# Layer 1's first product by seven products instead of eight, for two thirds of the tokens

## The chip, the core and the metric

One NeuronCore of one Trainium2 chip runs the whole program. Its engines are PE (TensorE, matrix products), DVE (VectorE), ACT (ScalarE), POOL (GpSimd) and SP, which here only issues DMA. The metric is the device time of one execution in microseconds (us); the median of several runs counts.

## The reference, cut to what matters

```python
# q, k, v: 4 x 8 heads x 576 x 64, fp32; Dmat: causal decay by head
ret = (q @ k.T / 8) * Dmat;  x = (ret @ v), rearranged to 2304 x 512
# layer 1: w_in 512 x 2048, w_out 2048 x 512
h = x @ w_in
g = np.where(h >= 1, h, np.where(h <= -1, 0, (h + 1) ** 2 / 4))
x = g @ w_out
# layer 2: w_a, w_b 512 x 1536, w_out 1536 x 512
out = ((x @ w_a) * (x @ w_b)) @ w_out
```

## The kernel before

Every fp32 operand x of the two layers is split in two: high = x rounded to the matrix engine's format by an ACT copy, low = x - high on DVE. A product is then three matmuls (high*high, high*low, low*high). Tokens are always along the free axis of `x_all` (4 blocks of 128 features x 2304 tokens), which stays in SBUF.

**Attention** (16 units of two heads) runs first and fills `x_all`. It is the only part in which POOL works.

**Layer 1** goes through the tokens in five tiles t of 512, 512, 256, 512 and 512 tokens (`WIDTHS`), and in each through 16 blocks f of 128 hidden features. `hidden(t, f)` is 12 matmuls (4 input blocks x 3) into a PSUM bank, and `project(t, f)` 12 more, which add the block's share of w_out to four banks `y_b`; PE runs `hidden(f)`, `project(f - 2)`. Between them stands `gate`: ACT takes two relus from PSUM (L893, L895), DVE adds and multiplies (L717, L720), ACT rounds (`gh`, L904), DVE takes the low part (`gl`, L726). The weights' split is made in tile 0 (`round_w1`, `split_w1`), three blocks ahead. In tiles 1 to 4, after the gates that `prep_steps` names, DVE and ACT also prepare layer 2's weights: four sums of 256 columns (`block_sums`), the rounding of seven operands (`round_ops`, L840 of 768 columns and L842 of 1,024) and their low parts (`split_ops`, L657, L660). SP stores them to DRAM, 12 blocks in all.

**Layer 2** has three tiles of 768 tokens with 12 steps u each. A step computes blocks of a = x w_a and b = x w_b by Strassen's scheme in Winograd's form: seven products of half-size operands instead of eight. A product is 6 matmuls of 384 columns. PE's order in a step (`step2`) is: product 1, product 2, product 7 of the step before, `rows` (three half-shares of the product with w_out, 6 matmuls of 512 columns each, from step 5 on), product 5, product 4 of the step before, product 6, product 3. ACT and DVE copy and add the products in between (u1, a0, b1, p5, u2, a1), DVE multiplies (`prod1`, and `prod0` once product 4 is done, L781), ACT rounds (`ph`, L946 and L957) and DVE takes low parts (`pl`). Product 1 of step u + 1 reuses the bank that `prod0` of step u - 1 has read, and so waits for `prod0_ready`, and for the step's weights, which SP loads into one of three buffers `wop` when product 4 of three steps before is done.

Every engine works through its own list in the written order; a semaphore wait holds all that stands behind it on that engine.

## Time and profile before

| | us |
|---|---|
| median of 3 runs | 881.57 (881.54 to 882.55) |
| the profiled execution | 882.61 |
| its span, first to last instruction | 880.1 |
| PE busy | 870.2 (99%) |
| DVE busy | 479.8 (55%) |
| ACT busy | 334.6 (38%) |
| POOL busy | 37.0 (4%), all in the attention part |
| granted TensorE clock, mean | 1.00 of full speed |

The profiled execution is 1.04 us above the median, and 2.5 us of it lie outside the span. Layer 1 starts on PE at 67.3 us of the span, layer 2's first product at 461.6 us. A matmul's busy time (390 ns for 512 columns) is longer than the distance to the next one (227 ns), since they are pipelined; how fast PE gets on is read from start to start.

### The profile page before, as it was taken

How to read it: one execution, taken by the hardware profiler on the slowest of the kernel's cores; microseconds unless marked ns; L12 is line 12 of the kernel's file. 1: busy time of each engine (PE TensorE's matmuls, PEld its weight loads, DVE VectorE, ACT ScalarE, POOL GpSimd, SP SyncE). 2: the span in 40 equal slices, each digit the busy share in tenths (PEclk: the TensorE clock that was granted, in tenths of full speed). 3: DMA queues.
4: the chain of work that ended last, by engine and by line, in shares of the span. 5: the costliest groups of instructions: out<-in, count | busy, mean ns of one | idle time of the engine just before them, and what ended most of it. 6: DMA issues, size and time to landing. Idle time of an engine off the chain costs nothing.

```text
span 880.1 us, 13001 instructions
## 1 busy us (share of the span) xinstructions
PE 870.2 (99%) x5232; PEld 777.0 (88%) x5232; DVE 479.8 (55%) x829; ACT 334.6 (38%) x598; POOL 37.0 (4%) x54
## 2 busy tenths in 40 slices
PE   7999999999999999999999999999999999999998
PEld 6998888888899888888889999999999999999996
DVE  4686665555656755665653533574433574534443
ACT  1235554444445544444443333342233242223220
POOL 4660000000000000000000000000000000000000
PEclk9999999999999999999999999999999999999999
...
GB/s 344 329 348 264 1 0 1 79 111 116 111 123 108 54 107 119 111 112 105 118 149 189 243 168 184 198 157 200 150 198 157 284 159 215 168 216 168 227 60 72
DMA packets 33451, 136.89 MB, mean 156 GB/s; under 512 B 2672, under 2 KB 13424, under 8 KB 28784
## 3 DMA queue, kind: packets, MB, share of 16 engines
...
q10 hardware_dynamic: 144, 0.20, 0.1%
...
## 4 chain that ended last, share of the span: by engine, by line
PE 97%; DMA 1%; SPq 1%; DVE 0%; ACT 0%; issue 0%; POOL 0%; POOLq 0%; DVEq 0%; ACTq 0%
PE score_b L523 6%; PE score_b L527 6%; PE score_b L525 6%; PE score_a L527 4%; PE score_a L523 4%; PE score_a L525 4%; PE score_a L477 4%; PE kv_b L494 4%; PE kv_b L496 4%; PE score_a L479 4%; PE ret_b L496 4%; PE score_b L479 4%; PE score_a L478 4%; PE kv_b L495 4%; PE score_b L477 4%; PE ret_b L495 4%
## 5 line engine op out<-in xcount | busy, mean ns | idle before, releaser
L717 DVE TENSOR_TENSOR gate_w<-relu_s,relu_r 128x512 f32<-128x512 f32 (+1 forms) x80 | 51.0, 638 | 97.2 <-ACT relu_r L895 97.1
L523 PE MATMUL score_b<-xop_hi,wop 128*128 128x384 f32 x288 | 96.8, 336 | 0.1
L527 PE MATMUL score_b<-xop_hi,wop 128*128 128x384 f32 x288 | 96.7, 336 | 0.0
L525 PE MATMUL score_b<-xop_lo,wop 128*128 128x384 f32 x288 | 96.5, 335 | 0.0
L904 ACT ACTIVATE gh<-gated 128x512 fp32r<-128x512 f32 (+1 forms) x80 | 47.2, 590 | 105.9 <-DVE gated L720 105.9
L726 DVE TENSOR_TENSOR gl<-gated,gh 128x512 fp32r<-128x512 f32 (+1 forms) x80 | 51.1, 639 | 50.8 <-ACT gh L904 50.6
L523 PE MATMUL score_a<-xop_hi,wop 128*128 128x384 f32 x216 | 72.2, 334 | 0.0
L527 PE MATMUL score_a<-xop_hi,wop 128*128 128x384 f32 x216 | 72.2, 334 | 0.0
L525 PE MATMUL score_a<-xop_lo,wop 128*128 128x384 f32 x216 | 72.2, 334 | 0.0
L954 ACT ACTIVATE p<-score_b 128x384 f32<-128x384 f32 x36 | 17.7, 490 | 105.3 <-PE score_b L527 105.3
L523 PEld LDWEIGHTS score_b<-xop_hi,wop 128*128 128x128 f32 x288 | 54.1, 188 | 2.0 <-ACT p L954 0.4
L946 ACT ACTIVATE ph<-prod 128x384 fp32r<-128x384 f32 x36 | 18.9, 526 | 96.4 <-DVE prod L763 96.4
L525 PEld LDWEIGHTS score_b<-xop_lo,wop 128*128 128x128 f32 x288 | 54.1, 188 | 1.3
L527 PEld LDWEIGHTS score_b<-xop_hi,wop 128*128 128x128 f32 x288 | 54.0, 188 | 0.0
L720 DVE SCALAR_TENSOR_TENSOR gated<-relu_s,gate_w 128x512 f32<-128x512 f32 (+1 forms) x80 | 51.1, 638 | 2.7
L781 DVE TENSOR_TENSOR prod<-score_a,a 128x384 f32<-128x384 f32 x18 | 10.0, 557 | 72.6 <-PE score_a L527 72.6
L893 ACT ACTIVATE relu_s<-score_a,half 128x512 f32<-128x512 f32 (+1 forms) x40 | 25.8, 646 | 55.4 <-PE score_a L479 55.4
L781 DVE TENSOR_TENSOR prod<-score_b,a 128x384 f32<-128x384 f32 x18 | 10.0, 557 | 64.5 <-PE score_b L527 64.5
L477 PE MATMUL score_a<-xh,w1a 128*128 128x512 f32 (+1 forms) x120 | 44.4, 370 | 0.0
L478 PE MATMUL score_a<-xl,w1a 128*128 128x512 f32 (+1 forms) x120 | 44.2, 368 | 0.0
L479 PE MATMUL score_a<-xh,w1a 128*128 128x512 f32 (+1 forms) x120 | 44.1, 368 | 0.0
L548 PE MATMUL kv_b<-wo_hi,pl 128*128 128x512 f32 x112 | 43.9, 392 | 0.0
...
## 6 DMA issues: line engine op xcount, KB each, us to landing
...
```

The costliest lines, as they stand in the source:

```text
L477: pe.matmul(o, w1_slab(f, 0)[:, at], xh[:, k, 0:WIDTHS[t]], start=(k == 0), stop=False)
L478: pe.matmul(o, w1_slab(f, 0)[:, at], xl[:, k, 0:WIDTHS[t]], start=False, stop=False)
L479: mm = pe.matmul(o, w1_slab(f, 1)[:, at], xh[:, k, 0:WIDTHS[t]], start=False, stop=(k == KT - 1))
L495: pe.matmul(o, w1_slab(f, 0)[:, at], gl[:, f % RING, 0:WIDTHS[t]], start=False, stop=False)
L496: mm = pe.matmul(o, w1_slab(f, 1)[:, at], gh[:, f % RING, 0:WIDTHS[t]], start=False, stop=(f == NF1 - 1))
L523: pe.matmul(o, w[:, 0, at], xop_hi[b][:, k, :], start=(start and k == 0), stop=False, skip_group_check=True)
L525: pe.matmul(o, w[:, 0, at], xop_lo[b][:, k, :], start=False, stop=False, skip_group_check=True)
L527: mm = pe.matmul(o, w[:, 1, at], xop_hi[b][:, k, :], start=False, stop=(k == 1), skip_group_check=True)
L717: nc.vector.tensor_tensor(gate_w[:, 0:WIDTHS[t]], relu_s[:, 0:WIDTHS[t]], relu_r[:, 0:WIDTHS[t]], ALU.add).then_inc(gatew_ready, 1)
L720: nc.vector.scalar_tensor_tensor(out=gated[:, 0:WIDTHS[t]], in0=relu_s[:, 0:WIDTHS[t]], scalar=1.0, in1=gate_w[:, 0:WIDTHS[t]], op0=ALU.mi ...
L726: nc.vector.tensor_tensor(gl[:, f % RING, 0:WIDTHS[t]], gated[:, 0:WIDTHS[t]], raw(gh[:, f % RING, 0:WIDTHS[t]]), ALU.subtract).then_inc(g ...
L904: nc.scalar.activation(gh[:, f % RING, 0:WIDTHS[t]], gated[:, 0:WIDTHS[t]], ACT.Copy).then_inc(gh_ready, 1)
```

## The change: what it does

- Layer 1's tokens 0 to 767 are still done by `hidden` and `project`, now in two tiles of 384 (`TC = 384`). The other 1,536 tokens form two tiles of 768, which run through the Strassen steps: a step v takes two of the 16 hidden blocks, so there are 8 steps a tile, v = 0 to 15. Layer 2 follows as steps v = 16 to 51 (u = v - 16).
- In such a step the four results a0, a1, b1 and the last main bank are hidden features before the gate. `gate_relu` (ACT) takes s = relu(h/2 + 1/2), `gate_sum` (DVE, two instructions) takes max(h, min(s, 1) s), `gate_high` (ACT) rounds, `low_parts` (POOL) takes the low part. There are four of each a step. The buffer `u_sum` serves both u1 and u2.
- The product with w_out is made of `chunk`s: 12 matmuls of 384 columns, four of them in one row in each of steps 3 to 18, between product 7 and product 5; DVE adds each to `x_all` (ACT copies the first of a tile).
- In layer 1's two ordinary tiles SP stores all split weights to DRAM (`store_slabs`), loads pairs of blocks once more (`load_s`), POOL makes the four sums, ACT and DVE split them after the gates in `prep_steps`, SP stores them (`store_s`). Steps 0 to 15 load their operands from there, and w_out's split.
- Layer 2's weights are no longer prepared in layer 1. In its first tile (u = 0 to 11) the operands of step u + 1 are made during step u in the buffer `wop` itself: POOL sums, `round_ops(u + 1, 0)` and `(u + 1, 1)` on ACT, `split_ops` on DVE. PE's product 1 waits for `op_lo_ready`, that is for both parts. SP stores them for the later tiles.

Three places in the engines' lists. First PE between steps 2 and 3 of layer 2 (products 3 and 1; product 4 of the step before and product 6 stand right ahead of them). `score_b` holds product 3's bank and, for an odd step, the main bank. Before:

```order
L523 MATMUL score_b<-xop_hi,wop 128x384 [waits p5_copied]
L525 MATMUL score_b<-xop_lo,wop 128x384
L527 MATMUL score_b<-xop_hi,wop 128x384
L523 MATMUL score_b<-xop_hi,wop 128x384
L525 MATMUL score_b<-xop_lo,wop 128x384
L527 MATMUL score_b<-xop_hi,wop 128x384
L523 MATMUL score_b<-xop_hi,wop 128x384 [waits wop_loaded0,prod0_ready]
```

After:

```order
L684 MATMUL score_b<-xop_hi,wop 128x384 [waits p5_copied]
L686 MATMUL score_b<-xop_lo,wop 128x384
L688 MATMUL score_b<-xop_hi,wop 128x384
L684 MATMUL score_b<-xop_hi,wop 128x384
L686 MATMUL score_b<-xop_lo,wop 128x384
L688 MATMUL score_b<-xop_hi,wop 128x384
L684 MATMUL score_b<-xop_hi,wop 128x384 [waits op_lo_ready,prod0_ready]
```

The matmuls are the same; the last row, product 1, waits for DVE's low parts in place of a load.

Second ACT in step 2 of layer 2 (u, u_sum: copies of the main bank; p: of product 5; ph: the roundings of the step's results; wo_hi: those of w_out). Before:

```order
L932 ACTIVATE u<-score_a 128x384 [waits p1_done,a0_ready]
L946 ACTIVATE ph<-prod 128x384 [waits prod1_ready]
L954 ACTIVATE p<-score_b 128x384 [waits p5_done,b1_ready]
L957 ACTIVATE ph<-prod 128x384 [waits prod0_ready]
L862 ACTIVATE wo_hi<-wo_raw 128x512 [waits wo_loaded0] x2
L965 ACTIVATE u<-score_a 128x384 [waits p6_done,a1_ready]
```

After:

```order
L1199 ACTIVATE u_sum<-score_a 128x384 [waits p1_done,a1_ready]
L1059 ACTIVATE wop<-ab_raw 128x768 [waits ab_loaded,op_stored0,p4_done]
L1216 ACTIVATE ph<-prod 128x384 [waits prod1_ready,rows_done]
L1227 ACTIVATE p<-score_b 128x384 [waits p5_done,b1_ready]
L1233 ACTIVATE ph<-prod 128x384 [waits prod0_ready]
L1062 ACTIVATE wop<-wop_sum 128x1024 [waits sums_ready]
L1098 ACTIVATE wo_hi<-wo_raw 128x512 [waits wo_loaded0] x2
L1244 ACTIVATE u_sum<-score_a 128x384 [waits p6_done,a0_ready]
```

Two roundings for step 3 have come in, the second (L1062) behind the rounding that waits for `prod0_ready`.

Third ACT in step 1, the second step of the stage that uses Strassen's scheme: before that is layer 2's, now layer 1's (x_all: the last ordinary tile's results). Before:

```order
L932 ACTIVATE u<-score_b 128x384 [waits p1_done,a0_ready]
L946 ACTIVATE ph<-prod 128x384 [waits prod1_ready]
L884 ACTIVATE x_all<-kv_b 128x512 [waits xl_ready,y_done]
L884 ACTIVATE x_all<-kv_b 128x512
L954 ACTIVATE p<-score_b 128x384 [waits p5_done,b1_ready]
```

After:

```order
L1199 ACTIVATE u_sum<-score_b 128x384 [waits p1_done,a1_ready]
L1182 ACTIVATE ph<-a_0 128x384 [waits g_ready]
L1182 ACTIVATE ph<-a 128x384 [waits g_ready]
L1173 ACTIVATE prod<-b,half 128x384 [waits g_ready,b1_ready]
L1182 ACTIVATE ph<-b 128x384 [waits g_ready]
L1127 ACTIVATE x_all<-kv_b 128x384 [waits xl_ready,y_done]
L1127 ACTIVATE x_all<-kv_b 128x384
L1227 ACTIVATE p<-score_b 128x384 [waits p5_done,b1_ready]
```

Three gate roundings and a relu stand ahead of the copy of product 5 (L1227), for which product 3 waits.

The diff, cut to its core:

```diff
-        prep_steps = {(1, 1): 0, (1, 5): 1, (1, 9): 2, (1, 13): 3, (2, 2): 4, (2, 8): 5,
-                      (3, 1): 6, (3, 5): 7, (3, 9): 8, (3, 13): 9, (4, 1): 10, (4, 5): 11}
+        prep_steps = {(0, 10): 0, (0, 12): 1, (0, 14): 2, (1, 0): 3, (1, 2): 4, (1, 4): 5, (1, 6): 6,
+                      (1, 8): 7}
+            for p in range(NF1 // 2):
+                load_s(p)
+                store_slabs(p)
+                if p:
+                    store_s(p - 1)
+            store_s(NF1 // 2 - 1)
+            for v in range(WBUF):
+                load_ops(v)
+            load_out1(0)
+            load_out1(1)
...
+            def store_slabs(p):
+                for f in (2 * p, 2 * p + 1):
+                    sp.wait_ge(w1_ready, f + 1)
+                    sp.dma_start(w1_outs[f // GROUP, :, :, f % GROUP, :],
+                                 raw(w1_all[f][:, :, DM:])).then_inc(slabs_stored, 16)
+                sp.dma_start(w1_ops[p, :, :, 0:2 * AW],
+                             raw(w1_all[2 * p][:, :, 0:2 * AW])).then_inc(slabs_stored, 16)
+                sp.dma_start(w1_ops[p, :, :, 2 * AW:3 * AW],
+                             raw(w1_all[2 * p + 1][:, :, AW:2 * AW])).then_inc(slabs_stored, 16)
+            def store_s(p):
+                sp.wait_ge(s_lo_ready, p + 1)
+                sp.dma_start(w1_ops[p, :, :, 3 * AW:], raw(s_op[p % 2][:, :, :])).then_inc(s_stored[p % 2], 16)
...
+            def load_ab(u):
+                if u:
+                    sp.wait_ge(op_lo_ready, 2 * u - 1)
+                    sp.wait_ge(sums_ready, 4 * u)
+                sp.dma_start(ab_raw[:, :], w2_ab[u]).then_inc(ab_loaded, 16)
+            def store_ops(u):
+                sp.wait_ge(op_lo_ready, 2 * u + 2)
+                sp.dma_start(w2_ops[u], raw(wop[(V1 + u) % WBUF][:, :, :])).then_inc(op_stored[u % WBUF], 16)
...
+            def sums(a11, a12, a21, a22, s1, s2, s3, s4, ready, n):
+                nc.gpsimd.tensor_tensor(s1, a21, a22, ALU.add).then_inc(ready, 1)
+                nc.gpsimd.tensor_tensor(s3, a11, a21, ALU.subtract).then_inc(ready, 1)
+                pool.wait_ge(ready, 4 * n + 1)
+                nc.gpsimd.tensor_tensor(s2, s1, a11, ALU.subtract).then_inc(ready, 1)
+                pool.wait_ge(ready, 4 * n + 3)
+                nc.gpsimd.tensor_tensor(s4, a12, s2, ALU.subtract).then_inc(ready, 1)
+            for p in range(NF1 // 2):
+                pool.wait_ge(s_loaded[p % 2], 16 * (p // 2 + 1))
+                a, o = s_raw[p % 2], s_sum[p % 2]
+                sums(a[:, 0, 0:AW], a[:, 0, AW:], a[:, 1, 0:AW], a[:, 1, AW:],
+                     *[o[:, i * AW:(i + 1) * AW] for i in range(4)], s_sums_ready, p)
+            def second_sums(u):
+                v = V1 + u
+                a11, a12, a22, a21 = [ab_raw[:, i * AW:(i + 1) * AW] for i in range(4)]
+                o = wop_sum[v % WBUF]
+                sums(a11, a12, a21, a22, *[o[:, (3 + i) * AW:(4 + i) * AW] for i in range(4)], sums_ready, u)
+            def low_parts(p, i):
+                half, row = [(0, 0), (1, 0), (1, 1), (0, 1)][i]
+                g = [a0[p % 2], a1, b1, prod1][i]
+                at, half = (2 * p + row) % GBUF, slice(half * HALF, (half + 1) * HALF)
+                pool.wait_ge(gh1_ready, 4 * p + i + 1)
+                nc.gpsimd.tensor_tensor(pl[at][:, half], g[:, :], raw(ph[at][:, half]),
+                                        ALU.subtract).then_inc(gl1_ready, 1)
+            for v in range(1, V1 + NF2):
+                if v <= V1:
+                    low_parts(v - 1, 0)
+                    low_parts(v - 1, 1)
+                if 0 <= v + 1 - V1 < NF2:
+                    second_sums(v + 1 - V1)
+                if v <= V1:
+                    low_parts(v - 1, 2)
+                    low_parts(v - 1, 3)
...
+                q, half, m = n // 8, n // 4 % 2, n % 4
+                pe.wait_ge(gl1_ready, 8 * q + 8)
+                pe.wait_ge(wo_loaded[q % 2], 32 * (q // 2 + 1))
+                if n < 4:
+                    pe.wait_ge(y_copied, KT * NT)
+                else:
+                    pe.wait_ge(rows_out[n % 4], n // 4)
+                o, at, tokens = y_b[n % 4][:, 0:HALF], slice(m * P, (m + 1) * P), slice(half * HALF, (half + 1) * HALF)
+                for i in range(GROUP):
+                    hi, lo = ph[(GROUP * q + i) % GBUF][:, tokens], pl[(GROUP * q + i) % GBUF][:, tokens]
+                    w_hi, w_lo = wo_hi[q % 2][:, i, at], wo_lo[q % 2][:, i, at]
+                    pe.matmul(o, w_hi, hi, start=(i == 0), stop=False)
+                    pe.matmul(o, w_hi, lo, start=False, stop=False)
+                    mm = pe.matmul(o, w_lo, hi, start=False, stop=(i == GROUP - 1))
+                mm.then_inc(rows_done, 1)
...
+                    if 0 <= u < NF2:
+                        pe.wait_ge(op_lo_ready, 2 * u + 2)
+                    else:
+                        pe.wait_ge(wop_loaded[v % WBUF], 16 * loads_of(v))
+                    product(1, v, main_b[v % 2], True).then_inc(p1_done, 1)
...
-                    pe.wait_ge(u2_copied, u)
-                    product(7, u - 1, main_b[(u - 1) % 2], False).then_inc(p7_done, 1)
-                for n, half in mine:
-                    rows(n, half)
-                if u < STEPS2:
-                    if u == 0:
+                    pe.wait_ge(u2_copied, v)
+                    product(7, v - 1, main_b[(v - 1) % 2], False).then_inc(p7_done, 1)
+                for n in chunks(v):
+                    chunk(n)
+                if u >= 0:
+                    for n, half in slots(u):
+                        rows(n, half)
...
+                    pe.wait_ge(u1_copied, v + 1)
+                    product(6, v, main_b[v % 2], False).then_inc(p6_done, 1)
+                    pe.wait_ge(p5_copied, v + 1)
+                    product(3, v, p5_b, False).then_inc(p3_done, 1)
...
+            def gate_sum(p, i):
+                s = [prod1, prod0, prod0, prod1][i]
+                h = [a0[p % 2][:, :], a1[:, :], b1[:, :], main_b[p % 2]][i]
+                o = [a0[p % 2], a1, b1, prod1][i]
+                dve.wait_ge(s_ready, 4 * p + i + 1)
+                nc.vector.scalar_tensor_tensor(out=s[:, :], in0=s[:, :], scalar=1.0, in1=s[:, :], op0=ALU.min,
+                                               op1=ALU.mult).then_inc(v_ready, 1)
+                dve.wait_ge(v_ready, 4 * p + i + 1)
+                nc.vector.tensor_tensor(o[:, :], h, s[:, :], ALU.max).then_inc(g_ready, 1)
...
+                if 0 <= u + 1 < NF2:
+                    split_ops(u + 1, 0)
+                move(v, 1)
+                add_chunks(v)
+                if u >= 0:
+                    add_rows(u, 0)
+                if gated_before:
+                    gate_sum(v - 1, 3)
+                elif v:
                     g = (u - 1) % GBUF
-                    dve.wait_ge(p4_done, u)
-                    nc.vector.tensor_tensor(prod0[:, :], main_b[(u - 1) % 2], a0[(u - 1) % 2][:, :],
+                    dve.wait_ge(p4_done, v)
+                    nc.vector.tensor_tensor(prod0[:, :], main_b[(v - 1) % 2], a0[(v - 1) % 2][:, :],
                                             ALU.mult).then_inc(prod0_ready, 1)
...
+                if 0 <= u + 1 < NF2:
+                    split_ops(u + 1, 1)
...
+            def round_ops(u, part):
+                v = V1 + u
+                o = wop[v % WBUF]
+                if part == 0:
+                    act.wait_ge(p4_done, v - WBUF + 1)
+                    if u >= WBUF:
+                        act.wait_ge(op_stored[u % WBUF], 16 * (u // WBUF))
+                    act.wait_ge(ab_loaded, 16 * (u + 1))
+                    nc.scalar.activation(o[:, 0, 0:3 * AW], ab_raw[:, 0:3 * AW], ACT.Copy).then_inc(op_hi_ready, 1)
+                else:
+                    act.wait_ge(sums_ready, 4 * u + 4)
+                    nc.scalar.activation(o[:, 0, 3 * AW:], wop_sum[v % WBUF][:, 3 * AW:],
+                                         ACT.Copy).then_inc(op_hi_ready, 1)
...
+            def gate_relu(p, i):
+                s = [prod1, prod0, prod0, prod1][i]
+                h = [a0[p % 2][:, :], a1[:, :], b1[:, :], main_b[p % 2]][i]
+                act.wait_ge([a0_ready, a1_ready, b1_ready, p4_done][i], p + 1)
+                if p and i < 2:
+                    act.wait_ge(gl1_ready, 4 * p)
+                elif i >= 2:
+                    act.wait_ge(g_ready, 4 * p + 2)
+                    if i == 3:
+                        act.wait_ge(gl1_ready, 4 * p)
+                nc.scalar.activation(s[:, :], h, ACT.Relu, bias=half[:, 0:1], scale=0.5).then_inc(s_ready, 1)
+            def gate_high(p, i):
+                half, row = [(0, 0), (1, 0), (1, 1), (0, 1)][i]
+                g = [a0[p % 2], a1, b1, prod1][i]
+                if p >= 4:
+                    act.wait_ge(rows_done, 8 * ((p - 4) // 2) + 8)
+                act.wait_ge(g_ready, 4 * p + i + 1)
+                nc.scalar.activation(ph[(2 * p + row) % GBUF][:, half * HALF:(half + 1) * HALF], g[:, :],
+                                     ACT.Copy).then_inc(gh1_ready, 1)
...
-                        act.wait_ge(a0_ready, u)
+                if gated_before:
+                    gate_relu(v - 1, 0)
+                    gate_relu(v - 1, 1)
+                if v < V:
+                    if v:
+                        act.wait_ge(a1_ready, v)
+                    act.wait_ge(p1_done, v + 1)
+                    nc.scalar.activation(u_sum[:, :], main_b[v % 2], ACT.Copy).then_inc(u1_copied, 1)
+                if gated_before:
+                    gate_high(v - 1, 0)
+                    gate_high(v - 1, 1)
+                if 0 <= u + 1 < NF2:
+                    round_ops(u + 1, 0)
+                if gated_before:
+                    gate_relu(v - 1, 2)
+                    gate_high(v - 1, 2)
...
+                if v < V:
+                    if v:
+                if gated_before:
+                    gate_relu(v - 1, 3)
+                    gate_high(v - 1, 3)
+                elif v:
                     act.wait_ge(prod0_ready, u)
                     nc.scalar.activation(ph[g][:, 0:HALF], prod0[:, :], ACT.Copy).then_inc(ph0_ready, 1)
-                    for v in outs_split(u):
-                if moving and f == 0:
-                    round_op(nxt, 6)
-            for u in range(STEPS2 + 1):
-                step2(u)
+                if 0 <= u + 1 < NF2:
+                    round_ops(u + 1, 1)
+                if u > 0:
+                    for w in outs_split(u):
+                        round_out(w)
+                if u >= 0:
+                    copy_rows(u, 1)
```

## Rows read from the trace of the kernel before

**Rows 1.** The page: busy time and instructions; the chain that ended last, by engine.
```profile
PE 870.2 (99%) x5232; PEld 777.0 (88%) x5232; DVE 479.8 (55%) x829; ACT 334.6 (38%) x598; POOL 37.0 (4%) x54
...
PE 97%; DMA 1%; SPq 1%; DVE 0%; ACT 0%; issue 0%; POOL 0%; POOLq 0%; DVEq 0%; ACTq 0%
```

**Rows 2.** Timeline of PE, layer 1: start us, us, line, operation.
```profile
80.59 0.39 PE L477 MATMUL score_b<-xh,w1a 128*128 128x512 f32 x1
...
83.31 0.39 PE L494 MATMUL kv_b<-gh,w1a 128*128 128x512 f32 x1
```

**Rows 3.** Timeline of PE, layer 2, around the end of product 4 of a step.
```profile
621.68 0.33 PE L523 MATMUL score_a<-xop_hi,wop 128*128 128x384 f32 x1
...
622.55 0.33 PE L527 MATMUL score_a<-xop_hi,wop 128*128 128x384 f32 x1
...
623.76 0.33 PE L523 MATMUL score_b<-xop_hi,wop 128*128 128x384 f32 x1
...
624.80 0.33 PE L523 MATMUL score_a<-xop_hi,wop 128*128 128x384 f32 x1
```

**Rows 4.** Timeline of DVE at the same place.
```profile
622.92 0.56 DVE L781 TENSOR_TENSOR prod<-score_a,a 128x384 f32<-128x384 f32 x1 [4.92 <-PE score_a L527]
```

**Rows 5.** Timeline of ACT at the same place.
```profile
623.52 0.53 ACT L957 ACTIVATE ph<-prod 128x384 fp32r<-128x384 f32 x1 [1.08 <-DVE prod L781]
623.95 0.62 ACT L862 ACTIVATE wo_hi<-wo_raw 128x512 fp32r<-128x512 f32 x1
```

**Rows 6.** Groups by line and shape, DVE: xcount, busy us, mean ns, idle before.
```profile
L720 DVE SCALAR_TENSOR_TENSOR gated<-relu_s,gate_w 128x512 f32<-128x512 f32 x64 | 44.3, 692 | 2.2
...
L792 DVE TENSOR_TENSOR a<-score_b,u 128x384 f32<-128x384 f32 x36 | 19.9, 553 | 13.1 <-PE score_b L527 12.6 <-ACT u L965 0.5
...
L660 DVE TENSOR_TENSOR op_lo<-op_sum,op_hi 128x1024 fp32r<-128x1024 f32 x12 | 14.7, 1226 | 0.0
...
L720 DVE SCALAR_TENSOR_TENSOR gated<-relu_s,gate_w 128x256 f32<-128x256 f32 x16 | 6.8, 425 | 0.5
```

**Rows 7.** Groups by line and shape, ACT.
```profile
L893 ACT ACTIVATE relu_s<-score_a,half 128x512 f32<-128x512 f32 x32 | 22.1, 690 | 51.5 <-PE score_a L479 51.5
...
L946 ACT ACTIVATE ph<-prod 128x384 fp32r<-128x384 f32 x36 | 18.9, 526 | 96.4 <-DVE prod L763 96.4
...
L842 ACT ACTIVATE op_hi<-op_sum 128x1024 fp32r<-128x1024 f32 x12 | 12.5, 1043 | 0.0
...
L893 ACT ACTIVATE relu_s<-score_a,half 128x256 f32<-128x256 f32 x8 | 3.8, 469 | 3.9 <-PE score_a L479 3.9
```

**Rows 8.** Timeline of PE, second step of layer 2 (step 1).
```profile
475.67 0.34 PE L527 MATMUL score_b<-xop_hi,wop 128*128 128x384 f32 x1
476.10 0.44 PE L523 MATMUL score_b<-xop_hi,wop 128*128 128x384 f32 x1
476.38 0.33 PE L525 MATMUL score_b<-xop_lo,wop 128*128 128x384 f32 x1
```

**Rows 9.** Timeline of ACT at the same place.
```profile
475.56 0.49 ACT L954 ACTIVATE p<-score_b 128x384 f32<-128x384 f32 x1
```

**Rows 10.** Timeline of POOL in the attention part.
```profile
44.90 0.86 POOL L396 TENSOR_TENSOR qd<-kq,decays 128x384 f32<-128x384 f32 x1 [1.44 <-PE ret_b L459]
...
63.51 1.70 POOL L396 TENSOR_TENSOR qd<-kq,decays 128x384 f32<-128x384 f32 x1 [1.12 <-PE ret_b L459]
65.17 0.30 POOL L400 TENSOR_TENSOR qd<-kq,decays 128x64 f32<-128x64 f32 x1
```

**Rows 11.** Timeline of DVE at the same place.
```profile
63.26 1.23 DVE L638 TENSOR_TENSOR w1a<-w1a_raw,w1a 128x1024 fp32r<-128x1024 f32 x1 [0.27 <-ACT w1a L834]
```

**Rows 12.** Window of layer 1: us, busy by engine, PE clock, DMA share, GB/s.
```profile
195.00:200.00 5.00, 5.00 (x23) 4.14 (x23) 1.64 (x4) 1.90 (x3) 0.00 (x0) 1.00 0.87 359
```

**Rows 13.** Windows at the start of layer 2.
```profile
472.00:474.00 2.00, 2.00 (x14) 2.00 (x13) 1.48 (x3) 0.00 (x0) 0.00 (x0) 1.00 0.99 377
...
478.00:480.00 2.00, 2.00 (x13) 2.00 (x12) 0.94 (x3) 0.49 (x1) 0.00 (x0) 1.00 0.99 423
```

494 lines of the change are left out of this document (280 added, 214 removed).

## The prediction

> **What bounds the kernel now.** I read the busy times first: PE is busy for 99% of the span, DVE for 55%, ACT for 38%, and the chain that ended last is 97% PE [rows 1]. So the kernel lasts as long as PE's list, and whatever makes PE wait is added in full. Next the starts of matmuls. In layer 1, 12 matmuls of 512 columns take from 80.59 to 83.31, 226.7 ns each [rows 2]; in layer 2, 12 of 384 columns take from 621.68 to 623.76, 173.3 ns each [rows 3]. The difference is 53.4 ns for 128 columns, 0.417 ns a column, which is the clock's upper level of 2.4 GHz; what stays is 13.3 ns for each matmul, whatever its width. A matmul of 256 columns then costs 120.0 ns. Last I looked at the joints, the places where PE goes on with what another engine has just made. The change puts new work into them. The joint that matters is the one from product 4 to the next product 1, with products 6 and 3 in between: product 4's last matmul starts at 622.55 and ends at t0 = 622.88, product 1 starts at 624.80, that is t0 + 1.92 [rows 3]. Until then PE needs nothing. DVE starts `prod0` 0.04 after t0 [rows 4], ACT rounds it 0.04 after its end and is free for its next operation at 623.95, t0 + 1.07 [rows 5]. Nothing waits there now. One joint of before does fail, in step 1: ACT ends the copy of product 5 at 476.05 [rows 9], PE's stream, due at 475.84, goes on with 476.10 and 476.38 [rows 8]. Its second matmul stands as if the first had started at 476.21, so from an engine's end to PE's stream it is 0.16, and that place costs 0.37.
>
> **The matmuls.** Before, layer 1 has 16 blocks x 24 matmuls x 5 tiles = 1,920: 1,536 x 0.2267 + 384 x 0.1200 = 394.3 us. After: two tiles of 384 columns, 768 matmuls; 16 steps x 42 for the seven products, 672; 64 chunks x 12, 768. That is 2,208 x 0.1733 = 382.7 us. The seven products save an eighth of the first product, 96 matmuls of 384 columns on 1,536 tokens, 16.6 us; the narrower matmuls give back 5. The stream gets shorter by **11.5 us**. Layer 2's and attention's matmuls stay.
>
> The Trainium skill ("TensorE: Matmul & The Clock Gate", Back-to-back issue gap) gives the distance of isolated matmuls at the upper clock as columns / 2.4 plus 2.5 ns; by that the narrower matmuls would give back only 0.7 us and the stream would shrink by 15.9 (an estimate from that page). The rows have 13.3 ns in place of 2.5, and they decide.
>
> **The joints of layer 2's first tile.** Here the operands of step u + 1 are made during step u. ACT's second rounding (1,024 columns, as L842: 1.04 us [rows 7]) stands behind the rounding of `prod0`, which waits for product 4. DVE's low part (as L660: 1.23 [rows 6]) waits for it, and product 1 waits for that. From t0: ACT is free at 1.07 [rows 5], rounds to 2.11, DVE from 2.15 to 3.38, PE goes on at 3.54. It wanted to at 1.92: a wait of 1.62. Nothing covers it, since between product 4 and product 1 PE has only products 6 and 3; rows and chunks stand ahead of product 4. Steps u + 1 = 2 to 11 have this joint: **10 x 1.62 = 16.2 us**.
>
> Steps 0 and 1 of layer 2 follow gates of layer 1, so the chain starts with the fourth gate: relu 384 columns wide (between 690 ns for 512 and 469 for 256 [rows 7]: 0.58), min-and-square (between 692 and 425 [rows 6]: 0.56), max (as an addition from PSUM, L792: 0.55 [rows 6]), each with a hop of 0.04: gate ready at t0 + 1.82. ACT rounds it (0.53 [rows 7]) and is free after 0.43, at 2.29, rounds the operands to 3.33, DVE ends at 4.60, PE goes on at 4.76. Wait 2.84, **2 x 2.84 = 5.7 us**.
>
> **The joints of layer 1's steps.** Product 1 of steps 4 to 15 waits only for the fourth gate: 1.82 + 0.16 = 1.98 against 1.92, 12 x 0.06 = **0.7 us**. Everything else of these steps (four relus, four roundings, three copies on ACT; fourteen or fifteen operations of about 0.55 us on DVE) has the four chunks to hide behind, 48 x 0.1733 = 8.3 us.
>
> Steps 1 and 2 have no chunks, only 7.3 us of matmuls each. In step 1 ACT reaches the copy of product 5 only after three gate roundings, a relu that waits for b1, and the copies of the last ordinary tile. Laid out with the durations above, b1 ends 3.9 us after the step's first matmul; the relu ends at 4.5. POOL's low part holds DVE's square until 4.7, max ends at 5.9, the rounding at 6.4, the two copies at 7.2, product 5's copy at 7.7. Product 3 was due at 6.2 and starts at 7.8: 1.6. The fourth gate then comes 0.65 too late for product 1. In step 2 the first relu waits for POOL's last low part of step 1, b1 is 1.05 late for product 4, product 5's copy 0.8 for product 3, the fourth gate 0.65 for product 1. Together **4.75 us**; from below I bound it by what the same place cost before, 0.4, from above by 8.2, if the four POOL operations of step 2, 0.86 each, hold DVE one after another. The 0.4 of before goes.
>
> **POOL.** A subtraction of 384 columns with both inputs in SBUF takes 0.86, one of 64 columns 0.30 [rows 10], so a sum of 256 about 0.65. POOL's work on layer 1's low parts hides behind the chunks; the sums of layer 2's operands for step u + 2 start at t0 and last 2.7. They collide: at 63.51 the same 0.86 operation took 1.70, and its end lies 0.72 after that of the 1,024-wide DVE subtraction that had started before it [rows 10, 11]. The reverse, DVE held by POOL, no row shows. It costs nothing at the least and one sum of 0.65 per joint at the most, 0 to 6.5 us over ten joints. I take 0.2 each, **2.0 us**, nearer to nothing, since only POOL's delay is in the rows.
>
> The rule for this is in the Trainium skill ("SBUF — State Buffer", Who interferes with whom): a DVE instruction with two SBUF inputs and a GpSimd instruction that reads SBUF exclude each other, and the one that started second waits for all of the first. The trace agrees for POOL's side. By the rule DVE's low part at t0 + 2.15 meets POOL's third sum: that is the second rival.
>
> **DMA in the ordinary tiles.** A step there is 24 x 0.1733 = 4.16 us. From block 10 of tile 0 on, each pair of steps (8.3 us) brings 1.83 MB of stored slabs, 1.05 MB of stored sums and 0.52 MB to load, 3.4 MB in all. The queue moved 359 GB/s at a share of 0.87 while storing [rows 12] and 377 to 423 at 0.99 while loading [rows 13], so I take 390: 8.7 us a pair. The queue falls behind by 0.4 each time, and the last sums reach ACT about 1 us late. PE has two half-steps, 4 us, in hand between a hidden block and its gate's use. I take 0. ACT's and DVE's loop there (two relus, gate, rounding, weights) is 3.9 us against 4.16.
>
> **The sum.** 882.61 - 11.5 - 0.4 + 16.2 + 5.7 + 0.7 + 4.75 + 2.0 = 900.1 for an execution like the profiled one. Median 1.04 lower: **899.0 us**.
>
> **The rivals.**
> 1. Forecast, the rounding between product 4 and product 1 binds twelve times: 893 to 905. For it: the order of ACT's list and the missing slack in rows 3 to 5. Chance 0.62.
> 2. POOL holds DVE as well, at nearly every joint. The third sum ends at t0 + 2.6 instead of the low part's start at 2.15, 0.45 more for ten joints instead of 0.2, and 2 more in steps 1 and 2: 903.5. For it: rows 10 and 11, seen from the other side; against it: no row of before has DVE held by POOL. Chance 0.20.
> 3. The stores bind. At 300 GB/s, below every row, a pair takes 11.4 us, 3.1 more than its steps; over five pairs 15, less 4 in hand: 11 more, 910. It decides from about 350 GB/s down. For it: the stores are pieces of 1 to 4 KB, and those of rows 12 are 7 KB. Chance 0.11.
> 4. Faster than before. The low part of the operands is ready by t0 + 1.92 (ACT takes it ahead of `prod0`'s rounding, or the time of a 1,024-wide operation overlaps with its neighbour). Then 16.2, 5.7 and 2.0 go and 875 is left. It decides once both stages together take less than 0.7 us after ACT is free; they take 2.3. Chance 0.05.
> 5. Gains and losses cancel: 0.02.
>
> About 0.2% is what a measurement of this kernel can tell from no change. Slower 0.93, faster 0.05, the same 0.02. The likeliest case alone spans 893 to 905. The range takes in the second rival and the lower edge of the third, and leaves the fourth out: 890 to 911.
>
> **What would show it.** In the trace after: 12 gaps of PE ahead of product 1 in layer 2's first tile, two of about 2.8 us and ten of 1.6 to 2.1, released by DVE's operand low part; none in the second and third tile. PE's matmuls in layer 1 sum to 382.7. Gaps ahead of product 3 in step 1 and of products 4 and 3 in step 2. Wrong are the joints if those gaps are missing or DVE was done long before; wrong is the DMA term if PE waits at the end of tile 0 or in tile 1, or step 0 starts later than 201 us into the span; wrong is the POOL term if L841 is 1.2 us long in each of them and starts right at ACT's end.

## The result and the profile after

The changed kernel takes 910.31 us (median of four runs, 909.31 to 910.35) against 881.59 (881.54 to 882.55): ratio 1.032, 95% interval 1.0302 to 1.0338. Slower, inside the range of 890 to 911, 11.3 us above the forecast of 899.0. Its profiled execution is the 909.31, with a span of 907.5 against 880.1; the other three took 1.0 us more, with spans of 908.5.

The page of the changed kernel, parts 1, 2 and 4, answers to [rows 1]:

```profile
PE 868.0 (96%) x5520; PEld 828.0 (91%) x5520; DVE 516.9 (57%) x873; ACT 348.0 (38%) x650; POOL 185.4 (20%) x198
...
PEclk9999999999999999999899999999999999999999
...
PE 80%; DVE 11%; ACT 5%; issue 2%; DMA 1%; SPq 1%; POOL 0%; ACTq 0%; DVEq 0%; POOLq 0%
```

PE has 288 instructions more, as forecast (2,208 less 1,920 matmuls), and DVE and ACT now hold 16% of the chain that was 97% PE. To see where, I took every start of a matmul and subtracted the start before it and the distance that a matmul of its width needs in a full stream (226.7 ns for 512 columns, 173.3 for 384). Before, what stays is 1.2 us in the whole span. After, it is 40.3. The span grew by 27.4, so the stream of matmuls itself shrank by 39.1 - 27.4 = 11.7 us (forecast 11.5). The loss is in six places. "Slow matmuls" are those that start 320 ns apart instead of 173, at the lower clock (last section). In this table a wait counts with the 0.1 us by which the matmul behind it is late too; elsewhere waits stand without it.

| place | forecast, us | measured, us |
|---|---|---|
| products 1 of steps 18 to 27 (ten joints) | 16.2 + 2.0 for POOL | 17.9 |
| product 1 of step 17 | 2.84 | 2.9 |
| product 1 of step 16 | 2.84 | 5.6, and 2.6 of slow matmuls behind it |
| steps 1 and 2 | 4.75 | 3.2, and 1.7 of slow matmuls |
| steps 4 to 15 | 0.7 | 0.6 |
| border from ordinary tile 0 to tile 1 | 0 | 5.3 |

An ordinary joint, timeline of PE, ACT, DVE and POOL around 478 us (start, duration, engine and line, operation, in brackets the idle time before it and who ended it); it answers to [rows 3 to 5]:

```profile
478.06 0.34 PE L688 MATMUL score_b<-xop_hi,wop 128*128 128x384 f32 x1
479.83 0.41 PE L684 MATMUL score_a<-xop_hi,wop 128*128 128x384 f32 x1 [1.43 <-DVE wop L841]
...
477.38 1.04 ACT L1062 ACTIVATE wop<-wop_sum 128x1024 fp32r<-128x1024 f32 x1
...
478.46 1.23 DVE L841 TENSOR_TENSOR wop<-wop_sum,wop 128x1024 fp32r<-128x1024 f32 x1 [0.54 <-ACT wop L1062]
...
478.47 1.79 POOL L522 TENSOR_TENSOR wop_sum<-wop_sum,ab_raw 128x256 f32<-128x256 f32 x1
```

This is the chain that was laid out: ACT's rounding of 1,024 columns, DVE's low part, PE 0.14 after it. PE starts 1.60 us late; the forecast was 1.62. Here POOL's sum is the one that waits: it began 0.01 after DVE's 1.23 and took 1.79.

The joint into step 16, PE, ACT, DVE and POOL:

```profile
435.67 0.34 PE L688 MATMUL score_b<-xop_hi,wop 128*128 128x384 f32 x1
441.17 0.66 PE L684 MATMUL score_a<-xop_hi,wop 128*128 128x384 f32 x1 [5.16 <-issue]
...
433.96 0.58 ACT L1173 ACTIVATE prod<-score_a,half 128x384 f32<-128x384 f32 x1 [0.49 <-PE score_a L688]
438.34 0.52 ACT L1182 ACTIVATE ph<-prod 128x384 fp32r<-128x384 f32 x1 [3.79 <-DVE prod L947]
438.77 1.04 ACT L1062 ACTIVATE wop<-wop_sum 128x1024 fp32r<-128x1024 f32 x1
...
428.68 1.49 DVE L837 TENSOR_TENSOR wop<-ab_raw,wop 128x768 fp32r<-128x768 f32 x1
430.14 3.13 DVE L848 TENSOR_TENSOR xop_lo<-x_all,xop_hi 128x768 fp32r<-128x768 f32 x2
433.30 2.02 DVE L862 TENSOR_TENSOR x_all<-x_all 128x768 f32<-128x768 f32 x2
435.24 1.01 DVE L888 TENSOR_TENSOR x_all<-kv_b,x_all 128x384 f32<-128x384 f32 x2
436.18 1.01 DVE L888 TENSOR_TENSOR x_all<-ret_b,x_all 128x384 f32<-128x384 f32 x2
437.10 0.55 DVE L944 SCALAR_TENSOR_TENSOR prod<-prod 128x384 f32<-128x384 f32 x1
...
439.84 1.23 DVE L841 TENSOR_TENSOR wop<-wop_sum,wop 128x1024 fp32r<-128x1024 f32 x1 [1.60 <-ACT wop L1062]
...
430.73 1.73 POOL L551 TENSOR_TENSOR pl<-b,ph 128x384 fp32r<-128x384 f32 x1
```

The relu of the fourth gate is done at 434.54 and DVE takes it up at 437.10, 2.6 us later: it is still making the next tile's x operands and adding chunks. The chain that was laid out then follows (4.07 us from DVE's start to PE's, laid out 4.10), and PE's next matmul behind the one of 435.67 starts at 441.17, 5.3 us late. Part of DVE's queue is POOL's doing: the low parts of 768 columns take 1.49 and 3.13 for two beside POOL, where one alone takes 0.95. That is about 1.8 us of the 2.6, an estimate from these rows.

The border of the ordinary tiles, PE, then DVE, then POOL:

```profile
134.13 0.41 PE L638 MATMUL score_a<-xh,w1a 128*128 128x384 f32 x1 [2.65 <-DVE xl L818]
...
122.60 1.23 DVE L823 TENSOR_TENSOR w1b<-w1b_raw,w1b 128x1024 fp32r<-128x1024 f32 x1 [0.39 <-ACT w1b L1044]
123.75 1.76 DVE L829 TENSOR_TENSOR s_op<-s_sum,s_op 128x1024 fp32r<-128x1024 f32 x1
125.44 1.09 DVE L912 TENSOR_TENSOR gate_w<-relu_s,relu_r 128x384 f32<-128x384 f32 x1
126.56 0.97 DVE L915 SCALAR_TENSOR_TENSOR gated<-relu_s,gate_w 128x384 f32<-128x384 f32 x1
...
132.90 4.10 DVE L818 TENSOR_TENSOR xl<-x_all,xh 128x384 fp32r<-128x384 f32 x4
...
122.92 1.50 POOL L519 TENSOR_TENSOR s_sum<-s_raw 128x256 f32<-128x256 f32 x1 [30.21 <-DMA s_raw<-w]
124.39 1.72 POOL L520 TENSOR_TENSOR s_sum<-s_raw 128x256 f32<-128x256 f32 x1
```

DVE's operations of 1.23 and 0.55 us take 1.76, 1.09 and 0.97 beside POOL's sums, and the four low parts of x, beside the next pair's sums, 4.10 in all, where four in a row take 1.97 in run 7. That is the side of the collision that no row of before had: DVE held by POOL.

### The profile page after: what moved, and what is told of

Same layout as the page of the kernel before. It is cut to its first block, busy times and chain, and to the rows that moved or that the text cites. A ratio compares the mean times of both kernels' runs of the same rounds, so it can differ in the third digit from the quotient of the medians.

```text
span 907.5 us, 14103 instructions
## 1 busy us (share of the span) xinstructions
PE 868.0 (96%) x5520; PEld 828.0 (91%) x5520; DVE 516.9 (57%) x873; ACT 348.0 (38%) x650; POOL 185.4 (20%) x198
## 4 chain that ended last, share of the span: by engine, by line
PE 80%; DVE 11%; ACT 5%; issue 2%; DMA 1%; SPq 1%; POOL 0%; ACTq 0%; DVEq 0%; POOLq 0%
PE score_b L684 7%; PE score_b L688 7%; PE score_b L686 7%; PE score_a L684 6%; PE score_a L686 6%; PE score_a L688 6%; PE kv_b L724 3%; PE kv_b L725 3%; PE kv_b L723 3%; PE ret_b L724 3%; PE ret_b L725 3%; PE ret_b L723 3%; PE kv_b L705 2%; PE kv_b L707 2%; PE kv_b L706 2%; PE ret_b L707 2%
## 5 line engine op out<-in xcount | busy, mean ns | idle before, releaser
L684 PE MATMUL score_b<-xop_hi,wop 128*128 128x384 f32 x416 | 140.9, 339 | 12.6 <-DVE wop L841 10.7
L688 PE MATMUL score_b<-xop_hi,wop 128*128 128x384 f32 x416 | 140.0, 337 | 0.0
L686 PE MATMUL score_b<-xop_lo,wop 128*128 128x384 f32 x416 | 139.7, 336 | 0.0
L684 PE MATMUL score_a<-xop_hi,wop 128*128 128x384 f32 x312 | 106.7, 342 | 12.9 <-DVE wop L841 7.4
L688 PE MATMUL score_a<-xop_hi,wop 128*128 128x384 f32 x312 | 105.7, 339 | 0.0
L684 PEld LDWEIGHTS score_b<-xop_hi,wop 128*128 128x128 f32 x416 | 78.4, 189 | 17.4 <-issue 12.4
L1227 ACT ACTIVATE p<-score_b 128x384 f32<-128x384 f32 x52 | 25.5, 491 | 153.5 <-PE score_b L688 153.5
L688 PEld LDWEIGHTS score_b<-xop_hi,wop 128*128 128x128 f32 x416 | 78.3, 188 | 0.0
L944 DVE SCALAR_TENSOR_TENSOR prod<-prod 128x384 f32<-128x384 f32 x64 | 38.0, 594 | 65.0 <-ACT prod L1173 65.0
L684 PEld LDWEIGHTS score_a<-xop_hi,wop 128*128 128x128 f32 x312 | 59.5, 191 | 15.8 <-issue 14.3
L688 PEld LDWEIGHTS score_a<-xop_hi,wop 128*128 128x128 f32 x312 | 59.7, 191 | 0.0
L686 PEld LDWEIGHTS score_a<-xop_lo,wop 128*128 128x128 f32 x312 | 59.6, 191 | 0.0
L551 POOL TENSOR_TENSOR pl<-a,ph 128x384 fp32r<-128x384 f32 x32 | 35.5, 1128 | 84.4 <-ACT ph L1182 84.4
L961 DVE TENSOR_TENSOR a<-score_a,u_sum 128x384 f32<-128x384 f32 x52 | 28.9, 555 | 26.9 <-PE score_a L688 26.3
L724 PE MATMUL kv_b<-wo_lo,ph 128*128 128x512 f32 x112 | 43.9, 392 | 0.0
L848 DVE TENSOR_TENSOR xop_lo<-x_all,xop_hi 128x768 fp32r<-128x768 f32 x35 | 35.1, 1021 | 15.0 <-ACT xop_hi L1088 14.8
L723 PE MATMUL kv_b<-wo_hi,ph 128*128 128x512 f32 x112 | 43.6, 389 | 0.0
## 6 DMA issues: line engine op xcount, KB each, us to landing
wo_lo<-w_outs SPq DMA_DIRECT2D x8, 1024.0 KB, 11.7
```

The source lines that it names most:

```text
L551: nc.gpsimd.tensor_tensor(pl[at][:, half], g[:, :], raw(ph[at][:, half]), ALU.subtract).then_inc(gl1_ready, 1)
L684: pe.matmul(o, w[:, 0, at], xop_hi[b][:, k, :], start=(start and k == 0), stop=False, skip_group_check=True)
L686: pe.matmul(o, w[:, 0, at], xop_lo[b][:, k, :], start=False, stop=False, skip_group_check=True)
L688: mm = pe.matmul(o, w[:, 1, at], xop_hi[b][:, k, :], start=False, stop=(k == 1), skip_group_check=True)
L723: pe.matmul(o, hi, w_hi, start=(u % GROUP == 0), stop=False)
L724: pe.matmul(o, hi, w_lo, start=False, stop=False)
```

## The experiments

Ten kernels. "The change" is the kernel at 910.3; "border" is that of ordinary tiles 0 and 1; waits of PE are read off as above. The time of a single run stands without an interval; its span less its waits and slow matmuls is 866.8 to 868.1 us in all ten and 867.2 in the change, so the lists of waits account for the times. Runs 5 to 8 were timed beside one execution of the kernel before of 883.8 us, 2 us above its usual time, so between them and the change a difference of 1 or 2 us says nothing by itself, and the waits in the traces decide.

**1. Both second parts early.** `round_ops(u + 1, 1)` behind `round_ops(u + 1, 0)`, on DVE likewise.

```diff
                 if 0 <= u + 1 < NF2:
                     round_ops(u + 1, 0)
+                    round_ops(u + 1, 1)
...
-                if 0 <= u + 1 < NF2:
-                    round_ops(u + 1, 1)
```

> Both second-part operations of layer 2's operands (ACT's rounding of the four sums, DVE's low part of them) stand right behind those of the first part, ahead of the chunks and rows, instead of between product 4 and product 1. Theory A (the place in ACT's and DVE's lists makes the joints; the sums themselves are ready early in the step): the eleven gaps of 1.6 to 2.9 us ahead of product 1 go (17.9 + 2.9 us), the one into step 16 shrinks from 5.3 to about 3.7, since DVE's 1.15 us now stand ahead of the preparation of the next x operands there: about 888 us, 885 if the clock no longer falls behind that gap. Theory B (the sums of POOL or the load of ab_raw are what comes late): ACT waits at the new place, the copy of product 5 behind it is late, and PE waits at product 3 instead: 905 or more.

892.7 us (four runs, 892.3 to 893.5), 1.0124 of before (1.0107 to 1.0141). Of the waits into steps 17 to 27 one of 1.4 us is left (the fourth gate's, into step 17), so the place in the lists did make them. But into step 16 PE waits 6.3, and in step 19 product 3 waits 1.2. ACT in step 15:

```profile
425.31 0.84 ACT L1058 ACTIVATE wop<-ab_raw 128x768 fp32r<-128x768 f32 x1
429.62 1.06 ACT L1061 ACTIVATE wop<-wop_sum 128x1024 fp32r<-128x1024 f32 x1 [3.47 <-POOL wop_sum L524]
430.58 0.60 ACT L1172 ACTIVATE prod<-b,half 128x384 f32<-128x384 f32 x1
```

That is theory B in part, and why 888 was missed by 5 us: in six of the twelve steps ACT stands at POOL's sums for 1.4 to 3.5 us, and in three of them PE waits for it. In step 15 the third relu comes 4.6 us later than in the change (425.99). I had taken the sums to be ready early in every step.

**2. Only ACT's rounding early.**

> Only ACT's rounding is moved ahead, DVE's low part stays between product 4 and product 1. If the chain is the sum of both stages, as the prediction put it, ACT's 0.95 and the rounding of prod0 ahead of it go from the path and DVE's list is left: prod0, the low part of prod1, the low part of the operands end at t0 + 2.2, PE goes on at t0 + 2.35 against 1.92. Ten gaps of 0.4 us instead of 1.7, the one into step 17 about 1.2 instead of 2.9, the one into step 16 about 3.9: some 16 us less than the changed kernel, 894. If DVE alone is the bound, little changes (908); if ACT alone, the gaps vanish (888).

899.4 us. The ten ordinary joints fall into two kinds: five of 0.40 to 0.45, as worked out, and five of 1.2 to 1.5. One of each, DVE, then POOL beside the first:

```profile
493.09 1.76 DVE L841 TENSOR_TENSOR wop<-wop_sum,wop 128x1024 fp32r<-128x1024 f32 x1
...
501.61 1.22 DVE L841 TENSOR_TENSOR wop<-wop_sum,wop 128x1024 fp32r<-128x1024 f32 x1
...
492.70 1.06 POOL L520 TENSOR_TENSOR wop_sum<-ab_raw 128x256 f32<-128x256 f32 x1
493.73 1.70 POOL L522 TENSOR_TENSOR wop_sum<-wop_sum,ab_raw 128x256 f32<-128x256 f32 x1
```

With POOL's sums at its side the low part of prod1 takes 0.78 instead of 0.55 and the operands' 1.76 instead of 1.22: 0.8 us a joint, against 0.3 in the change. The rest of the 5 us above the expected 894 is in steps 16 and 17: PE waits 6.0 and 1.6 there, not 3.9 and 1.2, since ACT stands at POOL's sums as in run 1 (3.5 us in step 15).

**3. Step 15's preparation behind the gate.**

```diff
+            if v == V1 - 1:
+                return {0: [], 1: [(j + 1, "op", 1)],
+                        2: [(j + 1, "op", 2), (j + 1, "t", 2), (j + 1, "t", 4), (j + 1, "op", 3)]}[place]
```

> In step 15 the x operand 2 and the two last differences of the next tile are made behind the step's last sum instead of ahead of the fourth gate. Theory A (DVE's backlog of this preparation makes the gap into step 16 5.3 us instead of the forecast 2.8, and the clock falls because the gap is that long): DVE starts the fourth gate's min-and-square at ACT's end, the gap is 2.8 us, and the 2.8 us of slow matmuls behind it go: 905. Rival (POOL's and DVE's collision at 430 makes it): the gap stays over 4 us: 909.

909.4 us, not the expected 905. The wait into step 16 is 2.81 us, so DVE's queue made the rest of the 5.3. The rival as it was put falls: DVE's operations ahead of the gate are still held by POOL (1.49 and 1.44), yet the gate starts on time. But together with the preparation the run took away one operation that POOL had held (1.76), and what the preparation would cost without POOL no run shows. The slow matmuls didn't go either: 9 behind this wait, 10 each behind two later ones (2.85 and 2.00) and 9 at the border. Waits and slow matmuls together are 40.3 us in both profiles: 3.8 less at this place, 1.5 and 1.9 more at the two later waits, 0.4 more at the border.

**4. ACT's order in steps 1 and 2.** Product 5's copy and the fourth relu ahead of the third gate's rounding, the tile's copies at the end of step 1.

> In steps 1 and 2 ACT copies product 5 and does the fourth relu ahead of the third gate's rounding, and the copies of the last ordinary tile stand at the end of step 1. Theory A (ACT's order makes the gaps of step 1 and 2): the gaps ahead of products 3 and 1, 3.2 us in all, shrink to 0.5 or less, and with them goes the fall of the clock from 221.7 to 225.5 (1.9 us): about 905.5. Rival (b1 is late because POOL's low parts hold DVE): the gaps ahead of product 3 go, those ahead of product 1 stay at 0.5 each, and the clock falls all the same: 908.

908.2 us. The waits ahead of products 3 and 1 are gone in both steps. In step 2 one of 1.3 us stands ahead of product 4:

```profile
225.79 0.44 PE L684 MATMUL score_b<-xop_hi,wop 128*128 128x384 f32 x1 [1.13 <-DVE b L969]
```

The forecast had it (b1 1.05 late); in the change the slow matmuls stand in its place, in runs 1 to 3 it is there with 1.3. The slow matmuls of step 1 are missing too, but they are missing in runs 1 to 3, which have the same waits there, so this run doesn't show why they came.

**5. Second parts placed behind the sums,** with the edit of run 3. In steps 15 and 16 they stand behind the third gate's rounding, in the others, on ACT, behind the copy of product 5 and, on DVE, ahead of `prod0`.

```diff
                     nc.scalar.activation(p5[:, :], p5_b, ACT.Copy).then_inc(p5_copied, 1)
+                if 1 < u + 1 < NF2:
+                    round_ops(u + 1, 1)
```

> The second part of layer 2's operands is made where its sums have just come: in the two steps that follow gates of layer 1 behind the third gate's rounding, in the other ten behind the copy of product 5 (ACT) and ahead of prod0 (DVE). Step 15's preparation of the next x operands is cut as in the run before that moved it. The run with both early parts left three waits (6.3 us into step 16, 1.4 into step 17, 1.2 in step 19) and 2.5 us of slow matmuls. If they come from ACT standing at POOL's sums, too far ahead in its list, they go, and the first layer-2 tile has no wait over 0.5 us: 882. If the early place itself is what the gates can't bear (DVE's 1.15 us ahead of the fourth gate), the waits into steps 16 and 17 stay at 1 to 1.5: 885.

898.1 us, with 28.2 us of waits and slow matmuls against 23.2 in run 1. The wait into step 16 is 1.1, but product 3 of step 16 waits 2.1 and product 1 of step 17 2.7, and the ten ordinary joints are back with 0.4 to 1.1 each (6.7 us), now released by `prod0`:

```profile
502.68 0.44 PE L687 MATMUL score_a<-xop_hi,wop 128*128 128x384 f32 x1 [0.93 <-DVE prod L999]
...
500.93 1.23 DVE L844 TENSOR_TENSOR wop<-wop_sum,wop 128x1024 fp32r<-128x1024 f32 x1 [1.11 <-ACT wop L1067]
502.07 0.55 DVE L999 TENSOR_TENSOR prod<-score_a,a 128x384 f32<-128x384 f32 x1
```

The low part has only changed places with the work it delayed. Both theories of this run (882 and 885) were too simple.

**6. The third pair's sums a tile later.** `prep_steps = {(0, 10): 0, (0, 12): 1, (1, 1): 2, (1, 3): 3, ... (1, 11): 7}`.

> Only two pairs' sums are rounded and split in the first ordinary tile (blocks 10 and 12), the other six from block 1 of the second tile on. Theory P (the place: the third pair's rounding and low part stand on ACT and DVE directly ahead of the next tile's x): 2.1 us less ahead of the x tile's rounding, and the wait at the border, 2.8 us, shrinks to about 0.8; POOL's sums still meet DVE there, so the small waits behind it (1.5 us) and the one at the copies (0.9) stay in part: 3 us less, 907. Theory L (POOL's sums hold DVE, three operations of 0.6 to 1.2 us took 1.1 to 1.8): the border loses at least 4 us still: 909. Theory D (the DMA queue): no change: 910.

912.0 us. The border's wait falls from 2.81 to 0.86, as theory P has it. DVE's first operations there are as long as in the change, but the low parts of x, now ahead of the next pair's sums, take 2.50 for four instead of 4.10, so the place and the collision both moved. The later pairs now come late, and ACT stands at the stored slabs:

```profile
182.68 0.85 ACT L1087 ACTIVATE xop_hi<-x_all 128x768 fp32r<-128x768 f32 x1 [6.76 <-DMA w_ops<-w1b]
```

PE waits 3.3 us at 184, with 1.7 of slow matmuls behind it, and 1.2 at 204. Here, not in the change, the stores bind.

**7. POOL's sums 8 columns wide.**

```diff
+                if ready is s_sums_ready and n >= 2:
+                    a11, a12, a21, a22, s1, s2, s3, s4 = [t[:, 0:8] for t in (a11, a12, a21, a22, s1, s2, s3, s4)]
```

> POOL's four sums of pairs 2 to 7 of layer 1's operands are 8 columns wide instead of 256; ACT and DVE round and split a piece of x_all of the same size in their place. This kernel leaves these sums out of the result. Every wait, transfer and operation of the other engines stays. Theory L: DVE's operations at the border go back to 0.55 and 1.23 us and the four low parts of x from 1.02 to 0.55 each: the border costs under 1.5 us instead of 5.3: 906. Theory P: the first wait stays over 2 us, only the small ones go: 908.5. Theory D: nothing changes: 910.

906.4 us. DVE at the same place:

```profile
124.22 1.23 DVE L831 TENSOR_TENSOR s_op<-s_sum,s_op 128x1024 fp32r<-128x1024 f32 x1
125.38 0.55 DVE L915 TENSOR_TENSOR gate_w<-relu_s,relu_r 128x384 f32<-128x384 f32 x1
125.96 0.56 DVE L918 SCALAR_TENSOR_TENSOR gated<-relu_s,gate_w 128x384 f32<-128x384 f32 x1
...
131.88 1.97 DVE L820 TENSOR_TENSOR xl<-x_all,xh 128x384 fp32r<-128x384 f32 x4
```

Every duration is back, and the border costs one wait of 0.7 us instead of 5.3 in all. The number and order of all operations, the sizes of those on ACT and DVE, and the transfers are the same. In the change ACT doesn't stand at the third pair's sums either (they end at 128.1, its rounding starts at 130.7), so it isn't their earlier end that helps here. Theory L holds.

**8. Thin stores.**

```diff
+                    wide = DM if f < GROUP else 8
                     sp.dma_start(w1_outs[f // GROUP, :, :, f % GROUP, 0:wide],
```

> The stores of W_out's rounded slabs are 8 columns wide from the fifth slab on, and the seven-product stage loads the first four slabs each time: 0.79 of 3.4 MB a pair less to write. This kernel's result is that of the wrong slabs. Theory D (the queue binds at the border): the sums reach ACT early, the border's 5.3 us go, 905. Theories P and L: the sums come earlier, but ACT's and DVE's lists and POOL's share of the port stay, so the border still costs 2 us or more, with the collision at another place: 907 to 910.

909.7 us. Window 120 to 130 us of the change, then of this kernel (us, busy time of PE, weight load, DVE, ACT and POOL, granted clock, DMA share, GB/s):

```profile
120.00:130.00 10.00, 10.00 (x60) 10.00 (x59) 7.94 (x10) 4.82 (x8) 5.12 (x4) 1.00 1.02 355
```

```profile
120.00:130.00 10.00, 10.00 (x59) 10.00 (x58) 7.94 (x11) 4.83 (x8) 4.94 (x4) 1.00 0.82 254
```

The queue now has a fifth of its time free, but POOL's sums start no earlier (123.3, in the change 122.9), the same DVE operations are held, and the first wait at the border is 3.1 us (2.8 in the change). Theory D falls.

**9. All causes together.** The edits of runs 1, 3 and 4; POOL makes the sums ahead of the first two low parts; two chunk additions behind the fourth gate in steps 15 and 16; relus 0 and 1 take each other's scratch; pairs 2 to 7 at (1, 0), (1, 1), (1, 3), (1, 5), (1, 7), (1, 8).

> The causes taken away together. Layer 2's second operand part is rounded and split behind the first one (as in the first run), and POOL makes layer 2's sums ahead of the gates' first two low parts, so that ACT doesn't stand at them in steps 15 and 16; step 15's preparation is cut, and two of the four chunk additions of steps 15 and 16 stand behind the fourth gate; steps 1 and 2 have ACT's other order, with relu 0 no longer behind POOL; the third pair's sums are rounded in the second ordinary tile. From the run with both parts early (892.7): its waits into steps 16 and 17 and the slow matmuls behind them (6.6 + 2.5 + 1.4) shrink to about 1.5, the border's 5 (with slow matmuls) to 1.5, steps 1 and 2's 4.5 to 1: 877, faster than the kernel before, whose 881.9 the matmuls alone undercut by 11.5. If POOL's early sums hold DVE's gates at steps 15 and 16 instead, 3 us stay there: 880. If the gains of the stream are not there in full, 885.

886.3 us (six runs, 883.7 to 887.3), 1.0045 of before (1.0031 to 1.006), 9 us above what was expected. 17.7 us of waits and slow matmuls are left. The large ones are at 181 (3.5), since ACT stands at the last pair's sums, and in step 16 (1.5 at 448, 2.8 at 451, 2.0 of slow matmuls behind):

```profile
179.73 1.06 ACT L1052 ACTIVATE s_op<-s_sum 128x1024 fp32r<-128x1024 f32 x1 [5.03 <-POOL s_sum L526]
...
438.56 1.58 ACT L1092 ACTIVATE xop_hi<-x_all 128x768 fp32r<-128x768 f32 x2 [3.01 <-DVE x_all L864]
```

**10. The two places mended.** The diff is against run 9; DVE's chunk additions in step 16 also move behind the fourth gate.

```diff
+            if v == V1:
+                return {1: [(j, "op", 5)], 2: [(j, "op", 6)], 3: [(j, "op", 3), (j, "op", 4)]}.get(place, [])
...
-        prep_steps = {..., (1, 0): 2, (1, 1): 3, (1, 3): 4, (1, 5): 5, (1, 7): 6, (1, 8): 7}
+        prep_steps = {..., (0, 15): 2, (1, 0): 3, (1, 2): 4, (1, 4): 5, (1, 6): 6, (1, 8): 7}
```

> As the run with all causes taken away together (886.3), with two places mended. The third pair's sums are rounded and split behind block 15 of the first ordinary tile, directly behind the next tile's x, and the later pairs where the change has them; in that run they stood a block later and ACT stood 5.0 us at POOL's sums of the last pair, PE 3.5 and 1.2 us behind it. And in step 16 ACT's relus stand ahead of the rounding of x operands 3 and 4 (ACT had waited 3.0 us there for DVE's differences), DVE's low part of operand 5 and all chunk additions stand behind the fourth gate. If the late sums make the waits at 181 and 203, both go (4.8 us); if ACT's wait for the differences makes those at 448 and 451, 1.5 and 2 of 2.8 us go and the slow matmuls behind them (2.0): 877 to 879, faster than the kernel before (881.8). If the waits are DVE's own load in step 16 (14.7 us of work for 15.6), 2.5 us stay there: 880. If the DMA queue binds once the sums come earlier: 884.

880.02 us (eleven runs, 879.0 to 882.6) against 881.92 (fifteen): ratio 0.998, 0.9971 to 0.9989. Faster than the kernel before, by 0.2%. The page:

```profile
PE 861.0 (98%) x5520; PEld 824.3 (94%) x5520; DVE 517.4 (59%) x873; ACT 347.1 (40%) x650; POOL 181.3 (21%) x198
...
PEclk9999999999999999999999999999999999999999
```

No matmul is slow in the profiled execution, and 10.9 us of waits are left, the largest 1.7 us at the copies of the ordinary tile (143) and 1.4 in step 16. With 878.3 of span, 880.1 - 11.7 + (10.9 - 1.2) is met within 0.2. The step at 181 is gone, the one at 202 (1.2) is not: half of that expectation. In step 16 waits of 1.4 and 1.0 stay, as the rival had it that DVE's own load makes them (2.5); no run tells it from another cause.

## Why the prediction was right, and where it was short

- **The number.** The median lies 0.7 us inside the range, and the likeliest case (893 to 905) is missed by 5. The range reached to 911 only for the second and third rivals, and the third isn't what happened: that the measured time is inside is in part luck. The other three executions, 1.0 us longer than the profiled one, had a granted clock of 0.992 against 0.994, which would fit more slow matmuls; they have no profile.
- **The matmuls.** 11.5 forecast, 11.7 measured. The width-free 13.3 ns of [rows 2, 3] holds. The estimate beside it, by the formula of the Trainium skill ("TensorE: Matmul & The Clock Gate", Back-to-back issue gap), is added up wrongly: 96 x 384 / 2.4 ns = 15.4 us fewer columns, less 288 x 2.5 ns = 0.7 for the matmuls added, is 14.6 us, not 15.9. The measured 11.7 is below either, and decides.
- **The joints.** Right in mechanism, place and size: ten at 1.6 to 1.9 us, one at 2.9, released by DVE's L841, none in the later tiles. Run 1 removed them. A joint that POOL leaves alone costs 1.67 with the matmul behind it, ten of them 16.7. POOL's share, 2.0 forecast, is 4 x 0.3 = 1.2: in four joints DVE's low part took 1.52 instead of 1.22.
- **The joint into step 16** is the first term that was mis-sized: "2 x 2.84". It is 5.6, and 2.6 for the clock. The step that failed is "the chain starts with the fourth gate": DVE was not free for that gate, because the x operands of the next tile are prepared in just this step, two of their low parts beside POOL; run 3 took the 2.5 us away. I had counted DVE's queue in steps 1 and 2, not here.
- **The border** is the second: "I take 0" for DMA, and "ACT's and DVE's loop there is 3.9 us against 4.16". The DMA part was right (run 8). The loop was counted with undisturbed durations; with POOL beside it DVE needs from 123.75 to 127.53 for three operations that take 2.3 (124.22 to 126.52) in run 7, and the third pair's rounding stands ahead of x. Runs 6 and 7 show that either one's removal takes 4.1 us or more of the 5.3, so the two add up at one place. The prediction's own sign, "wrong is the DMA term if PE waits at the end of tile 0" or step 0 starts after 201 us, came true (205.2), and pointed at the wrong term: in run 7, with the transfers unchanged, step 0 starts at 201.3.
- **The second rival** named the right mechanism at the wrong place. DVE is held by POOL, at little cost in the joints and, together with the third pair's rounding, at 5 us at the border, where POOL's sums had been counted only for when they end. The Trainium skill ("SBUF — State Buffer", Who interferes with whom) has this rule, and that a DVE instruction with at most one SBUF input, outside DVE's two-port modes, is free of it. The groups of the change agree with both: means of the DVE operations with both inputs in SBUF rise (L912 628 ns where 0.55 us is its undisturbed time, L848 1021 where it is 0.95), those with one input in PSUM don't (L961 555, L888 550 and 552), though 21 of the 52 of L961 ran beside POOL, none longer than 0.56 us.
- **Steps 1 and 2.** 4.75 forecast. Where the clock doesn't fall there (runs 1 to 3, 5 to 8) the five waits laid out are all there, 1.4, 0.6, 1.4, 0.7 and 0.7 us, 4.8 in all. In the change 1.7 us of slow matmuls stand in place of the third.
- **The clock** was in no term. In the profiled execution 28 matmuls are at the lower level, 320 ns apart instead of 173, and cost 4.3 us.

The two places above the forecast, 5.4 at step 16 and 5.3 at the border, less 0.7 elsewhere, are the 10 us by which the span missed (27.4 measured, 17.5 forecast). The third rival, 910, came out at the measured time, but by another cause.
